# Remaking the engine orders of an attention and two-MoE kernel: new load costs in the planner, VectorE scaling the first batch's coarse probabilities, block steps first on ScalarE

## The reference, cut to what matters

```
q_d = q.reshape(B, H, 144, 4, D).mean(axis=3)     # k_d, v_d likewise: groups of 4 tokens
out_up = repeat(softmax(scale * q_d @ k_d.T) @ v_d, 4)        # coarse part, 144 x 144 scores a head
mask = abs(pos[:, None] - pos[None, :]) < 4
out_local = softmax(where(mask, scale * q @ k.T, -1e9)) @ v   # band of 7 keys a token
x = (out_up + out_local) as (2304 tokens, 512)
x = (s * relu(x @ w_in)**2 + b) @ w_out                       # MoE 1, 512 -> 2048 -> 512
h = x @ w_in2;  y = (h - tanh(h)) @ w_out2                    # MoE 2, same sizes
```

## Time and profile before

| | us |
|---|---|
| three runs | 892.18, 893.32, 893.84 |
| median of the three | 893.32 |
| profiled execution, its own time | 892.53 |
| its span in the trace | 890.7 |
| PE busy in the span | 876.7 |
| DVE, ACT, POOL busy | 592.2, 467.4, 362.7 |

### The profile page before, as it was taken

The page is one execution under the profiler, slowest core; times in us unless marked ns, Lnnn a source line. Parts: engine busy times, 40 slices in busy tenths (PEclk is TensorE's granted clock), DMA queues, the critical chain, the costliest instruction groups (busy, mean ns, idle before and its releaser), DMA issues.

```text
span 890.7 us, 15923 instructions
## 1 busy us (share of the span) xinstructions
PE 876.7 (98%) x5956; PEld 824.6 (93%) x5956; DVE 592.2 (66%) x799; ACT 467.4 (52%) x1144; POOL 362.7 (41%) x348
## 2 busy tenths in 40 slices
PE   7999999999999999999999999999999999999997
PEld 6889999999999999999999998988899888998896
DVE  5658599989999999985213377677734447444444
ACT  2899575567545754545565454444533336333332
POOL 5567473966489663433732100022221315212120
PEclk8999999999999999999999999999999999999999
DMA  8971453353333323202102250110601001310012
GB/s 219 277 247 46 120 147 85 106 128 94 97 94 88 88 46 72 71 1 79 56 28 65 80 181 24 27 45 25 189 25 44 29 24 48 95 43 29 24 49 71
DMA packets 57904, 73.57 MB, mean 83 GB/s; under 512 B 19110, under 2 KB 36068, under 8 KB 57828
## 3 DMA queue, kind: packets, MB, share of 16 engines
q1 hardware_dynamic: 56233, 72.12, 29.3%
q10 hardware_dynamic: 1595, 0.43, 0.2%
HBM read 63.10 MB, written 9.44 MB: 81 GB/s over the span
## 4 chain that ended last, share of the span: by engine, by line
PE 92%; DVE 3%; ACT 2%; DMA 1%; issue 1%; SPq 1%; POOL 0%; ACTq 0%; DVEq 0%; POOLq 0%
PE acc L2226 23%; PE hid L2198 22%; PE hid L2263 19%; PE acc L2280 14%; PE pa L2280 7%; PE pa L2156 1%; PE pa L2123 1%; PE pa L1998 1%; DMA dkey<-in_k_dram 1%; PE pa L2140 1%; DVE x2l L1610 1%; PE pa L2169 1%; PE acc L1990 1%; DVE sum L1655 0%; PE hid L2206 0%
## 5 line engine op out<-in xcount | busy, mean ns | idle before, releaser
L1248 POOL TENSOR_TENSOR gl<-relu,gh 128x288 fp32r<-128x288 f32 x128 | 128.3, 1005 | 171.1 <-PE acc L2226 119.5
L2226 PE MATMUL acc<-gh,wbh 128*128 128x288 f32 (+1 forms) x512 | 154.5, 302 | 0.0
L2198 PE MATMUL hid<-xh,wah 128*128 128x288 f32 x512 | 153.5, 301 | 0.3 <-ACT relu L1886 0.2
L2226 PE MATMUL acc<-gl,wbh 128*128 128x288 f32 (+1 forms) x512 | 151.5, 296 | 0.0
L2226 PE MATMUL acc<-gh,wbl 128*128 128x288 f32 (+1 forms) x512 | 151.2, 295 | 0.0
L2198 PE MATMUL hid<-xh,wal 128*128 128x288 f32 x512 | 150.4, 295 | 0.0
L2198 PE MATMUL hid<-xl,wah 128*128 128x288 f32 x484 | 142.0, 294 | 0.0
L1886 ACT ACTIVATE relu<-hid 128x288 f32<-128x288 f32 x128 | 52.3, 408 | 129.9 <-PE hid L2198 107.6
L2263 PE MATMUL hid<-x2h,wqh 128*128 128x384 f32 x336 | 113.2, 337 | 2.4 <-DVE odd L1646 2.4
L2263 PE MATMUL hid<-x2h,wql 128*128 128x384 f32 x336 | 113.2, 337 | 0.0
L2263 PE MATMUL hid<-x2l,wqh 128*128 128x384 f32 x336 | 112.8, 336 | 0.0
(11 more groups left out here) (210 smaller groups left out, 1863.7 us busy)
## 6 DMA issues: line engine op xcount, KB each, us to landing
w2b_raw<-in_moe_w_out_dram SPq DMA_DIRECT2D x24, 512.0 KB, 3.6
kl<-in_k_dram SPq DMA_DIRECT2D x23, 240.0 KB
vl<-in_v_dram SPq DMA_DIRECT2D x23, 240.0 KB
x2T<-ystage SPq DMA_DIRECT2D x8, 576.0 KB, 3.2
own<-in_q_dram SPq DMA_DIRECT2D x11, 384.0 KB
wa_raw<-in_moe_w_in_dram SPq DMA_DIRECT2D x4, 1024.0 KB, 8.8
wb_raw<-in_moe_w_out_dram SPq DMA_DIRECT2D x4, 1024.0 KB, 10.4
x2raw<-x2T SPq DMA_DIRECT2D x10, 384.0 KB, 3.9
```

What stands on the lines that cost most here:

```text
L1248: g.tensor_tensor(out=gl[:, turn % LRING1, 0:NS], in0=relu[:, f % 2, :], in1=gh[:, turn % GRING1, 0:NS].bitcast(F32), op=ALU.subtract).the ...
L2198: one = pe.matmul(dst, w[:, group, d, cols], x[:, j % XRING, d, :], start=i == 0, stop=i == 3 * KT - 1)
L2226: one = pe.matmul(acc[:, d, n], w[:, f, cols], g[:, turn % ring, n], start=(f == 0 and p == 0), stop=(f == FT - 1 and p == 2))
```

## The change

Five costs of the planner's DMA model change, the blocks' `dense_exp` and `dense_place` get the lowest rank number on ACT (so they are taken first among steps that could start at the same time), and `score_scale` of batch 0 moves from ACT to DVE, as one instruction for both heads in place of two. All lists are then made anew.

```diff
+FIRST_PACKET, LANDING = 2.0, 1.5
 ...
-        dma_free, emptied, held = 0.0, [0.0, 0.0], set()
+        dma_free, emptied, held = FIRST_PACKET, [0.0, 0.0], set()
 ...
-                end = dma_free + 0.6
+                end = dma_free + LANDING
 ...
-            o.add("SP", 0.6, (2, 2 * g + 3 * i), (kind, g), after, kbytes=620)
+            o.add("SP", 0.6, (2, 2 * g + 3 * i), (kind, g), after, kbytes=690)
 ...
-        o.add("ACT", 0.5, (1, 0, 3 + 1), ("dense_exp", a), [("dense_max", a)])
+        o.add("ACT", 0.5, (-1, -1), ("dense_exp", a), [("dense_max", a)])
 ...
-        o.add("ACT", 0.8, (1, 0, 3 + 2), ("dense_place", a), [("dense_probs", a)]
+        o.add("ACT", 0.8, (-1, -1), ("dense_place", a), [("dense_probs", a)]
 ...
-                  kbytes=(240 if b else 200) if n < 6 else 180)
+                  kbytes=(240 if b else 300) if n < 6 else 175)
 ...
-            o.add("ACT", 0.64 * n, (0 if b else -1, b, rank + 1), ("score_scale", b, i), [("score_inverse", b, i)])
+            o.add("ACT" if b else "DVE", 0.64 * n if b else 0.5, (0 if b else -1, b, rank + 1), ("score_scale", b, i), [("score_inverse", b, i)])
 ...
+            elif kind == "score_scale":
+                b, i = key
+                ones = kept(b, i)
+                ve.wait_ge(s_sinv, step_count(b, i))
+                ve.tensor_tensor(pc[0:HG, ones, :], pc[0:HG, ones, :], over(cinv[0:HG, ones], [[1, 2], [0, GROUPS]]),
+                                 ALU.mult).then_inc(s_pc, 2)
```

More of the change, by code:

```diff
@@ L291, in plan @@
     for half in range(2):
[L293 to L296, removed]
+        o.add("SP", 1.6, (0, 0, half, 6), ("load_dense_keys", half), kbytes=360)
+    o.add("ACT", 2.5, (0, 0), ("load_first_queries",), kbytes=360)
+    o.add("SP", 1.6, (0, 0, 1, 6, 1), ("load_last_queries",), kbytes=360)
+    o.add("SP", 3.0, (1, 0, 0), ("load_dense_values",), kbytes=850)
     o.add("POOL", 3.0, (0, 1), ("dense_mask",))
@@ L318, in plan @@
     late = 1.0
-    for i, (kind, kbytes) in enumerate((("load_late_keys", 600), ("load_late_queries", 590), ("load_late_values", 870))):
+    for i, (kind, kbytes) in enumerate((("load_late_keys", 730), ("load_late_queries", 730), ("load_late_values", 850))):
         o.add("SP", (2.4, 1.8, 3.0)[i], (2, (1, 1, 4)[i], i), (kind,), kbytes=kbytes)
```

## The result

The changed kernel takes 896.41 us (median of 6 runs, 894.93 to 897.47); the kernel before takes 893.02 (6 runs, 892.18 to 893.84). The ratio is 1.0038, with an interval of 1.0028 to 1.0049: 3.4 us slower, where 890.3 was forecast. The profiled execution took 896.88 us over a span of 895.1, so the two profiled executions are 4.35 us apart.

What follows compares the result with a forecast made beforehand. PE, busy 876.7 of 890.7 us, was taken as the bound. The terms, -5.0 + 1.8 + 1.5 - 0.6 = -2.3 us, gave 890.2 against the profiled execution, named as 890.3; range 887.7 to 893.3.

Steps and rivals of the forecast that it cites:

- Term 2: Between `hidden1 0 0` and `hidden1 0 5`, PE newly waits after `hidden1 0 2`: +1.8 us, bounds +0.8 and +2.8.
- X: Start of the MoE work, `hidden1 0 0`: 43.31 us before the change, forecast near 38.3.
- Term 3: At the new PE wait after `hidden1 0 2`, the clock falls: +1.5 us, bounds 0 and +3.4.
- term 1: In the opening, `hidden1 0 0` starts earlier: -5.0 us, bounds -6.1 and -3.0.
- Rival 2: In the opening, three of VectorE's four scales meet POOL's additions, 0.62 us more each: 891.6 us, chance 0.18.
- Term 4: End of tile 0, PE's 0.41 us wait in a ring knot at 109.20: -0.6 us, bounds -1.0 and +0.6.
- Rival 3: From 9 us behind the start of `hidden1 0 0`, repeated ring waits keep the clock low: 895.7 us, chance 0.10.

Runs made afterwards that it cites:

- run 9: Changed kernel with 20 idle transposes ahead of `turn_probs 0 4`, inside PE's wait there: 893.24 us, ratio 1.0006 to the kernel before.
- run 3: Changed kernel's lists up to the planned start of `hidden1 0 0`, lists of the kernel before from there on: 892.42 us, ratio 0.9992.
- run 4: Lists of run 3, plus POOL's first two `w1_low` held until `dense_add 0` and `dense_add 3`: 890.82 us, ratio 0.9981.
- run 5: run 4 with the load `load_w1b 0` issued earlier, directly behind `load_w1a 0`: 888.09 us, ratio 0.9942.
- run 12: run 8 with POOL's first two `w1_low` held until `dense_add 0` and `dense_add 3`: 891.59 us, ratio 0.9983.
- run 8: Kernel before with only batch 0's `score_scale` moved to VectorE, all lists made anew: 893.64 us, ratio 1.0019, in two groups.
- run 2: Changed kernel with 20 more idle transposes ahead of `dense_values 2`: 893.60 us, ratio 1.0010 to the kernel before.
- run 11: Kernel before with only the new ranks of `dense_exp` and `dense_place` on ScalarE, all lists made anew: 893.09 us, ratio 1.0002.
- run 1: Changed kernel with POOL's first two `w1_low` held until `dense_add 0` and `dense_add 3`: 893.86 us, ratio 1.0006 to the kernel before.

## Why the prediction was wrong

**What held.** PEclk 1.00 through 17 to 23 us, `scores 0 0` at 22.91 (forecast 22.7). Term 2's place and kind: two waits ahead of `turn_probs` (2.33) and `late_turn` (0.93), released by `score_exp` and `place_probs`. `hidden1 0 3` at X + 12.2 (forecast 11.6). Term 3: a second fall, +1.5 forecast; run 9's profile gives 1.8.

**The step that failed** is in term 1: "the nearest rows are 0.45 us and 0.73 us on average, up to 1.07 while POOL adds groups", taken as bounds of -6.1 and -3.0. The fourth scale took 2.90, and term 1 came to -0.5 in place of -5.0. Rival 2 had the right mechanism but left out the partner that counts: it went by POOL's additions alone, which end "about when norm 3 starts". They ended at 32.90, just behind the start of the fourth scale, and then POOL began two `w1_low` in a row. The trace of before has a `dense_norm` product that ran beside a `w1_low` and took 0.72 instead of 0.50. This row was read only as part of an average:

```profile
31.97 1.27 POOL L1231 TENSOR_TENSOR wal<-wa_raw,wah 128x512 fp32r<-128x512 f32 x1
32.88 0.72 DVE L1353 TENSOR_TENSOR dprob<-dprob,dinv 128x330 f32<-128x330 f32 x1
```

What it does not have is the pair: the next `w1_low` came at 37.31. In the new lists the two stand together behind the additions. *The Trainium skill* (SBUF — State Buffer, Who interferes with whom) says that whichever of the two issues first gets the shared ports, for its whole instruction. By that, an estimate, the scale waits for the addition only, 0.13 + 0.45 = 0.6 us. The trace disagrees: the scale is recorded 0.09 us ahead of the first `w1_low` and waited for both, and in run 3 a product recorded 0.41 us ahead did the same.

**What the step set off** is the larger part: 2.08 us of idling, then half clock from 37.3 to 44.1 us. By run 4 these are 2.2 and 2.6 us up to the start. With the lock gone (runs 4 and 5) X is 38.08 and 37.60, so the rest of term 1's sum was right. Term 3 asked whether the clock falls in the new stall behind X and never whether it could fall ahead of it.

**Terms 2 and 3 together** were forecast at +3.3 and measured at +4.4: 65.67 - 61.32 + 0.5, less 0.4 for `weigh 0 6`, which was done later before. 0.6 of the rest stands ahead of `hidden1 0 3`.

**A second weak step stayed hidden.** Term 2 let the load of `w1_high 0 1` land at 41.6, "no more than 0.5 us of wait". In run 4, with the start at 38.08 and that step ahead of the relu, it was 4.12. In the changed kernel the late start covered the load.

**Term 4** was -0.6. The knot at 109.20 is gone, a wait of 0.4 us came at 91.55, and up to the start of tile 1 about -0.4 is left (3.55, less 4.35 - 0.4). Behind that the prediction counted nothing, and +0.8 came, most of it the wait of 0.7 at 210.37. That is a new wait beyond 120 us, one of its own signs of being wrong.

**The sum and the rivals.** The last step of the sum does not follow: 890.2 and the 0.8 by which the median lay above the profiled execution make 891.0, not 890.3. Rival 3's 895.7 is near the measured 896.41 by chance. Its mechanism, a clock held low by one ring wait after the other behind X + 9, is not what happened: of the two falls the first lies ahead of X, and PEclk is 1.00 from 58 to 894 us.

By parts of the change, each alone in the kernel before: ranks 0.1, load costs +2.3 (earlier start, worse order behind it), VectorE's scales -1.4 without the lock (run 12) and +4 or more in the executions with it. The gain was there, but an order that looks only at planned starts spent it.

## What to carry to other kernels

When an elementwise product with two SBUF inputs moves to VectorE, or when its lists shift, read POOL's rows at the microsecond in which each product will run. As the worst case price it by the whole run of POOL instructions that stand back to back there. It can be cheaper to hold POOL back than to look for another engine (run 12: 1.4 us under the kernel before, and a spread of 1.1 us where run 8 has 7.8).

A short wait of PE can cost its length and then the half clock behind it (2.2 and 2.6 us here). Where the wait can't be removed, idle transposes put into it can give the second part back (run 9: the second fall gone, 1.8 us between the profiled executions). Where the wait doesn't come in every execution, they can become the delay themselves (run 2's profile).

An earlier start is worth only what the next queue can take: after each fix ask which load now lands too late (run 4, then run 5).

## What was not expected of the hardware

- A VectorE product recorded while POOL's last addition ran was served only behind that addition and both `w1_low` that followed: 2.90 us in the changed kernel, 2.91 in run 8 and 2.90 in run 9 against 0.45, and 3.25 in run 3 against 0.50. With one `w1_low` behind the addition it was 1.93 (run 11).
- It is not always so. Of two `x_low` that met two `w1_low`, each waited for one of them (about 1.5 us each, 2.98 to 3.00 for both against 0.83; runs 1, 4, 5 and 12), and the second `w1_low` took 1.49 us instead of 1.26. What decides whether VectorE gets in between was not found.
- It is not only products. In run 2 a copy of 128x8 took 2.46 us beside the pair, against 0.16 otherwise.
- The same program can fall in two groups about 6 us apart, by whether one instruction meets such a pair (run 8, and run 12 without it).
- In the changed kernel, after 2.08 us of idling and 1.2 us of work, PEclk fell; it was back 6.8 us later, with PE busy throughout.
